# Four score tiles of head 1 brought forward ahead of head 0's last tile, with bias buffers of their own, and 24 identity turns behind them

## The reference, cut to what matters

```python
scores = q @ k.T / sqrt(64)
psi_rel = log1p(abs(pos[:, None] - pos[None, :])); psi_i = log1p(max(pos[:, None], 1))
bias = relu((psi_rel / psi_i)[..., None] @ w1 + b1) @ w2       # 576 x 576 x 8 heads
attn = softmax(scores + bias)
x = (attn @ v) of all heads as 2304 x 512
x = (s * relu(x @ w_in) ** 2 + b) @ w_out
out = (h - tanh(h)) @ w2_out, with h = x @ w2_in
```

## Time and profile before

| | |
|---|---|
| median of 3 runs | 1090.35 us (1090.28 to 1091.12) |
| the profiled execution, its own time | 1089.92 us |
| its span, first to last instruction | 1088.1 us |
| mean granted TensorE clock | 0.998 |
| busy: TensorE, VectorE, ScalarE, GpSimd | 97%, 57%, 67%, 63% |
| DMA, mean busy share by the queue of sync | 67.2% |

### The profile page before, as it was taken

One profiled execution on the slowest core, in us unless ns is written; L12 is line 12 of the kernel. 1 busy time (PEld: TensorE's weight loads), 2 busy tenths in 40 slices (PEclk: granted clock), 3 DMA queues, 4 the chain that ended last, 5 costly groups with the idle time before them and its releaser, 6 DMA issues.

```text
span 1088.1 us, 16872 instructions
## 1 busy us (share of the span) xinstructions
PE 1050.2 (97%) x5685; PEld 912.5 (84%) x5685; DVE 625.1 (57%) x1128; ACT 728.4 (67%) x1469; POOL 690.6 (63%) x656
## 2 busy tenths in 40 slices
PE   6679999999999999999999999999999999999998
PEld 2168889888888888888888888888888888999998
DVE  7968877655775475567747755761450451440640
ACT  8978888767878587777758766873562553552652
POOL 1056666687778778868876887766454455455553
PEclk9999999999999999999999999999999999999999
DMA  5788867799889788998996799764333333333331
GB/s 191 252 251 261 269 196 175 198 253 230 211 214 259 205 210 237 238 212 196 255 268 164 184 274 245 186 145 134 106 116 98 99 115 125 119 121 101 96 122 64
DMA packets 185338, 201.19 MB, mean 185 GB/s; under 512 B 125811, under 2 KB 129829, under 8 KB 185253
## 3 DMA queue, kind: packets, MB, share of 16 engines
q1 hardware_dynamic: 185108, 200.04, 67.2%
q10 hardware_dynamic: 144, 0.07, 0.1%
HBM read 155.23 MB, written 15.64 MB: 157 GB/s over the span
## 4 chain that ended last, share of the span: by engine, by line
PE 70%; ACT 14%; issue 7%; DVE 6%; DMA 2%; POOL 1%; SPq 0%; DVEq 0%; ACTq 0%; POOLq 0%
PE ps_f L919 19%; PE ps_f L921 19%; PE ps_f L920 19%; ACT x_raw L345 2%; PE ps_o L555 2%; DVE g_buf L979 2%; PE ps_s L594 2%; ACT planes L642 2%; ACT gh L932 2%; DVE g_buf L982 2%; PE ps_s L595 1%; PE ps_o L558 1%; PE ps_o L570 1%; ACT ps_t L654 1%; ACT gh L936 1%
## 5 line engine op out<-in xcount | busy, mean ns | idle before, releaser
L876 POOL TENSOR_TENSOR wl<-w_raw,wh 128x512 fp32r<-128x512 f32 x318 | 418.3, 1320 | 255.9 <-ACT wh L869 254.8
L919 PE MATMUL ps_f<-gh,wh 128*128 128x464 f32 (+1 forms) x640 | 242.7, 379 | 2.3 <-DVE g_buf L979 1.7
L919 PE MATMUL ps_f<-xh,wh 128*128 128x464 f32 (+1 forms) x640 | 240.5, 376 | 0.6 <-DVE ptl L748 0.6
L921 PE MATMUL ps_f<-xh,wl 128*128 128x464 f32 (+1 forms) x640 | 237.4, 371 | 0.0
L920 PE MATMUL ps_f<-gl,wh 128*128 128x464 f32 (+1 forms) x640 | 237.4, 371 | 0.0
L921 PE MATMUL ps_f<-gh,wl 128*128 128x464 f32 (+1 forms) x640 | 237.2, 371 | 0.0
L920 PE MATMUL ps_f<-xl,wh 128*128 128x464 f32 (+1 forms) x640 | 237.1, 370 | 0.0
L869 ACT ACTIVATE wh<-w_raw 128x512 fp32r<-128x512 f32 x318 | 196.6, 623 | 48.4 <-PE ps_f L921 48.2
L919 PEld LDWEIGHTS ps_f<-gh,wh 128*128 128x128 f32 x640 | 120.8, 189 | 16.0 <-DVE g_buf L979 2.8
L919 PEld LDWEIGHTS ps_f<-xh,wh 128*128 128x128 f32 x640 | 120.5, 188 | 13.4 <-DVE ptl L748 0.8
L921 PEld LDWEIGHTS ps_f<-xh,wl 128*128 128x128 f32 x640 | 120.1, 188 | 13.4
(11 more groups left out here) (126 smaller groups left out, 1694.8 us busy)
## 6 DMA issues: line engine op xcount, KB each, us to landing
w_raw<-in_w_out SPq DMA_DIRECT2D x80, 512.0 KB, 3.6
w_raw<-in_w_in SPq DMA_DIRECT2D x79, 512.0 KB, 3.5
bias_t<-bias_flat SPq DMA_DIRECT2D x128, 288.0 KB, 4.0
bias_flat<-stage SPq DMA_DIRECT2D x36, 295.5 KB, 2.2
k_raw<-in_kt SPq DMA_DIRECT2D x32, 288.0 KB, 4.1
q_raw<-in_qt SPq DMA_DIRECT2D x32, 288.0 KB, 3.6
v_raw<-in_vt SPq DMA_DIRECT2D x22, 288.0 KB, 3.2
bias_t<-bias_flat SPq DMA_DIRECT2D x32, 144.0 KB, 4.3
```

Of the source, the lines that this page charges most:

```text
L876: pool.tensor_tensor(wl[:, b % RING, :, :], raw_block(b), wh[:, b % RING, :, :].bitcast(F32), ALU.subtract).then_inc(w_lo_done, 1)
L919: pe.matmul(acc, hi, rhs_h[:, k0 + kk, 0:T], start=(first and kk == 0), stop=False)
L921: mm = pe.matmul(acc, lo, rhs_h[:, k0 + kk, 0:T], start=False, stop=(last and kk == 3))
```

## The change

Head 1's tiles 0 to 3 are scored, added and exponentiated in step 4, ahead of head 0's tile 4, and no longer in steps 5 to 8. Their bias goes to `early_bias`, four buffers which share their memory with `gl` (of the third stage), and is loaded right behind head 0's tile of the same t. The two banks go on alternating for these nine tiles. Sync then loads head 2's tiles 0 to 3 in steps 0 to 3 and nothing of the bias in steps 5 to 8. `neg_max` gets two halves by head. Head 1's q is rounded before step 0 and its low part taken at t = 0. The two weight blocks are rounded by ScalarE at g = 4 instead of 3, where GpSimd's low parts stay at g = 3. Behind step 4 TensorE does 24 turns of the identity into `ps_f`.

```diff
+PRE = 4
         def load_bias(sp, t):
...
             sp_bias(sp, 0, t)
+            if t < PRE:
+                sp_bias(sp, 1, t)
...
+        def scored_ahead(g):
+            if NT <= g < NT + PRE:
+                return g - 1
+            return NT + PRE - 1 if g == NT - 1 else g
+        def all_scored(n):
+            return NT + PRE if n == 0 else (n + 1) * NT
+        def scoring_at(g):
+            return g < TILES and not NT <= g < NT + PRE
         def score_bank(n, t):
-            if n == 0 and t % 2:
-                return ps_o
+            if n * NT + t < NT + PRE:
+                return ps_o if scored_ahead(n * NT + t) % 2 else ps_s
...
-            if n == 0:
-                need(pe, min_done, t - 1)
-                pe.wait_ge(back_done, PACKS - 2 if t == 0 else PACKS)
+            if n * NT + t < NT + PRE:
+                need(pe, min_done, scored_ahead(n * NT + t) - 1)
+                pe.wait_ge(back_done, PACKS - 2 if n + t == 0 else PACKS)
...
         def pe_turn(pe, i, alone):
             if t == 0:
-                pe.wait_ge(exp_done, (v + 1) * NT)
+                pe.wait_ge(exp_done, all_scored(v))
...
-            if t == 1 and n + 1 < BH:
+            if t == 1 and 0 < n < BH - 1:
                 act_round_q(act, n + 1)
...
-            if t == 1 and n + 1 < BH:
+            if t == (1 if n else 0) and n + 1 < BH:
                 pool_low_q(pool, n + 1)
...
         def sp_step(sp, g):
-            if n + 1 < BH:
-                sp.wait_ge(min_done, n * NT + t + 1)
-                sp_bias(sp, n + 1, t)
+            to = n + 1 if t >= PRE or n > 1 else 2 if n == 0 else BH
+            if to < BH:
+                sp.wait_ge(min_done, scored_ahead(g) + 1)
+                sp_bias(sp, to, t)
...
         @block.scalar
+            act_round_q(act, 1)
             for g in STEPS_AT[:FIRST]:
+                if g == NT - 1:
+                    for pre in range(NT, NT + PRE):
+                        act_exp(act, pre)
                 act_step(act, g, True)
-                if g == 3:
+                if g == NT - 1:
                     act_weights(act, 0)
                     act_weights(act, 1)
...
         @block.vector
+                if g == NT - 1:
+                    for pre in range(NT, NT + PRE):
+                        dve_add(dve, pre)
...
         @block.tensor
             for g in STEPS_AT[:FIRST]:
+                if g == NT - 1:
+                    for pre in range(NT, NT + PRE):
+                        pe_score(pe, *divmod(pre, NT))
+                if g == NT + PRE:
+                    pe.wait_ge(inv_row_done, 1)
                 pe_step(pe, g, True)
+                if g == NT - 1:
+                    pe_idle_turns(pe, ps_f, 24)
```

More of the change, by code:

```diff
@@ L123, in build @@
         v_loaded = sem("v_loaded")
+        early_loaded = [sem(f"early_loaded{i}") for i in range(PRE)]
         bias_loaded = [sem(f"bias_loaded{t}") for t in range(NT)]
@@ L200, in act_round_q @@
             act.wait_ge(q_loaded, (n + 1) * DMA)
-            need(act, s_done, (n - 1) * NT)
+            need(act, s_done, all_scored(n - 2) if n > 1 else 0)
             act.activation(q2[:, n % 2, 0:S], q_raw[:], ACT.Copy, scale=lower[:, 0:1]).then_inc(q_hi_done, 1)
@@ L205, in pool_round_k @@
             pool.wait_ge(k_loaded, (n + 1) * DMA)
-            need(pool, s_done, (n - 1) * NT)
+            need(pool, s_done, all_scored(n - 2) if n > 1 else 0)
             pool.tensor_copy(k2h[:, n % 2, :], k_raw[:]).then_inc(k_hi_done, 1)
@@ L217, in pool_low_k, with bias_home, bias_in @@
                 .then_inc(k_lo_done, 1)
+        def bias_home(n, t):
+            return early_bias[:, t, :] if n == 1 and t < PRE else bias_t[:, t, :]
+        def bias_in(eng, n, t):
+            if t >= PRE:
+                eng.wait_ge(bias_loaded[t], (n + 1) * DMA)
+            elif n == 1:
+                eng.wait_ge(early_loaded[t], DMA)
+            else:
+                eng.wait_ge(bias_loaded[t], max(n, 1) * DMA)
         def sp_bias(sp, n, t):
@@ L221, in sp_bias @@
             rows = bias_skew[P * t:P * t + R, bass.ds(n % H * PITCH + (S - 1), S)]
-            sp.dma_start(bias_t[0:R, t, :], rows).then_inc(bias_loaded[t], DMA)
+            loaded = early_loaded[t] if n == 1 and t < PRE else bias_loaded[t]
+            sp.dma_start(bias_home(n, t)[0:R, :], rows).then_inc(loaded, DMA)
         vhl = tile("vhl", [P, 2, NT, 2 * D], F32R)
@@ L230, in build @@
         o_tmp = tile("o_tmp", [D, 2, HALF])
-        neg_max = tile("neg_max", [P, NT])
+        neg_max = tile("neg_max", [P, 2, NT])
         den = tile("den", [P, 2, NT])
@@ L248, in build @@
         gh = tile("gh", [P, KF, TMAX], F32R)
+        with nc.sbuf_tensor("early_bias", [P, PRE, S], F32) as early_bias:
+            pass
         with nc.sbuf_tensor("gl_head", [P, KF - 2, TMAX], F32), nc.sbuf_tensor("p_odd", [P, S], F32) as p_odd:
@@ L620, in pe_step @@
                 pe_turn_inv(pe, n - 1)
-            if scoring(n):
+            if scoring_at(g):
                 pe_score(pe, n, t)
@@ L643, in act_plane, with act_exp @@
                 .then_inc(p_hi_done, 1)
+        def act_exp(act, g):
+            n, t = divmod(g, NT)
+            if t == 0:
+                need(act, den_done, min(n - 1, TURNED))
+            act.wait_ge(min_done, scored_ahead(g) + 1)
+            p = score_home(n, t)
+            act.activation(p, p, ACT.Exp, scale=-1.0, bias=neg_max[:, n % 2, t:t + 1],
+                           accum_out=den[:, n % 2, t:t + 1]).then_inc(exp_done, 1)
         def act_step(act, g, alone, between=None):
@@ L647, in act_step @@
             i, j = turned(g), valued(g)
[L649 to L655, removed]
             if j is not None and j % NT == NT - 1:
@@ L663, in act_step @@
                 act_plane(act, f)
-            if scoring(n) and alone and t == NT - 1:
-                exponential()
+            if scoring_at(g) and alone and t == NT - 1:
+                act_exp(act, g)
             if i is not None:
@@ L673, in act_step @@
                 between()
-            if scoring(n) and not (alone and t == NT - 1):
-                exponential()
+            if scoring_at(g) and not (alone and t == NT - 1):
+                act_exp(act, g)
             if n >= TURNED and between:
@@ L684, in act_step @@
                 need(act, inv_done, v)
-                act.wait_ge(exp_done, (v + 1) * NT)
+                act.wait_ge(exp_done, all_scored(v))
                 act.activation(den_e[:], den[:, v % 2, :], ACT.Copy, bias=1e-9).then_inc(den_done, 1)
-            if t == 1 and n + 1 < BH:
+            if t == 1 and 0 < n < BH - 1:
                 act_round_q(act, n + 1)
@@ L761, in dve_plane, with dve_add @@
                 .then_inc(p_lo_done, 1)
+        def dve_add(dve, g):
+            n, t = divmod(g, NT)
+            dve.wait_ge(s_done, scored_ahead(g) + 1)
+            bias_in(dve, n, t)
+            if t == 0 and n < TURNED:
+                need(dve, pt_done, (n - 1) * NT)
+            dve.tensor_tensor_reduce(out=score_home(n, t), in0=score_bank(n, t)[:, :, 0:HALF],
+                                     in1=halves(bias_home(n, t)), scale=-SCALE, scalar=3.0e38,
+                                     op0=ALU.add, op1=ALU.min, accum_out=neg_max[:, n % 2, t:t + 1])\
+                .then_inc(min_done, 1)
         def dve_step(dve, g, alone, between=None):
@@ L768, in dve_step @@
                 dve_scale(dve, f)
-            if scoring(n):
-                dve.wait_ge(s_done, g + 1)
+            if scoring_at(g):
+                dve.wait_ge(s_done, scored_ahead(g) + 1)
             if t == 3 and turning(n):
@@ L775, in dve_step @@
                 dve.tensor_copy(inv_row[:], ps_s[0:NT, 0, HALF:HALF + P]).then_inc(inv_row_done, 1)
[L776 to L783, removed]
+            if scoring_at(g):
+                dve_add(dve, g)
             if f is not None:
```

## The result

The changed kernel takes 1093.05 us (median of 22 runs, 1089.94 to 1096.59) against 1090.53 (22 runs of the kernel before, 1088.78 to 1092.49). The ratio is 1.0023, 95% interval 1.0018 to 1.0029. That is 2.5 us, just past the 0.2% that I had called distinguishable, and outside the range that I gave. The profiled execution took 1092.78 us with a span of 1091.0.

The account below looks back on a forecast made before the run. TensorE was taken to bound the steady stretch, DMA waits the passage. The q wait takes the offered 3.6 us, so (2,0) starts at 77.0 against 76.64: +0.4 on 1090.35, rounded to 1090.8 us; range 1088.7 to 1092.1.

Parts of the forecast that it names:

- The early loads in the tables: Table stage: three early bias loads between stores hidden to within 0.1 us, at most 1 us lost; put at 0.
- The load in front of the last stores: End of the tables: tile (1,3)'s load delays the last store and (0,4)'s bias by 0.8 us, bounds 0 to 1.0.
- Scores and additions in the gap: Passage to attention: four head 1 tiles fit into the bias wait, hiding 3.3 us, clock staying at 2.4 GHz.
- The 24 turns at 0.11 each, hidden: Behind step 4: turns take 2.6 us, ending at 68.7 before the first real turn at 68.75, costing nothing.
- ScalarE's wait for head 2's q: Step 6: q lands at 73.6, ScalarE waits 2.4 us, and the offered 3.6 us are gone.
- The shift stays: From head 2's first score on, the TensorE-bound loop carries the passage's +0.4 us to the end.
- Rival (c): Table stage: stalled stores hold ScalarE up some 0.6 us at each of three places, +1.8 us, 1092.6; 5%.
- (a): Passage: head 2's q comes soon enough, four shorter steps pay, (2,0) starts at 74 to 74.5, 1088.0 us; 12%.
- (b): Behind step 4: turns at 0.21 us each end at 71.1 and the slow clock holds on, +2.5, 1092.9 us; 5%.
- (d): Passage: the gap is merely filled, everything after stands as before, 1090.4 us; counted inside the forecast's 78%.

Follow-up runs that it names:

- Run 1: The kernel before plus only the change's bias buffers and early loads of head 1's tiles 0 to 3, no reordered scoring or turns: 1093.48 us, ratio 1.0026.
- run 3: The changed kernel without the 24 turns: 1093.07 us, ratio 1.0025.
- run 4: The changed kernel with head 2's k and q issued right behind bias (0,4), ahead of head 2's bias tiles: 1090.98 us, ratio 1.0003.
- Run 6: The changed kernel with only three tiles of head 1 loaded and scored ahead, so no load in front of the last two stores: 1092.25 us, ratio 1.0018.
- run 2: The changed kernel without its four early loads; head 1's first four tiles take head 0's bias: 1090.72 us, ratio 1.0005.
- run 10: The kernel of run 2 with head 2's k and q also issued right behind bias (0,4): 1089.71 us, ratio 0.9992.
- run 12: The kernel of run 9 without the 24 turns: 1092.66 us, ratio 1.0016.
- run 5: The changed kernel with head 1's bias tiles 0 to 2 loaded four packs behind head 0's and tile 3 behind bias (0,4): 1093.33 us, ratio 1.0030.
- run 8: The kernel of run 5 with head 2's k and q also issued early, after tile 3: 1093.26 us, ratio 1.0025.
- run 7: The kernel before with only head 2's k and q issued right behind bias (0,4), ahead of head 1's bias tiles: 1092.48 us, ratio 1.0019.
- run 9: The changed kernel with three early loads, four packs later, head 1's k and q at packs 11 and 15, head 2's behind bias (0,4): 1090.45 us, ratio 0.9997.

## Why the prediction was wrong

I forecast +0.4 us and 1090.8; it is +2.5 and 1093.05. By the steps of the prediction:

- **The early loads in the tables, "I put 0": this step failed.** I had written that the first place is hidden to within 0.1 us and priced the excess as a rival at 5%. The profile shows 0.6 us lost at pack 14, 0.3 at pack 22 and 0.2 at pack 30, 1.0 in all (tables 51.74 against 50.74), and 1.6 to 2.4 us in the profiles of runs 1, 3, 4 and 6, which have the same three loads. The four profiles with the old loads in the tables spread over 0.5 us, so the 1.0 of this one is rough, but the waits for the stage buffer name the place. The arithmetic missed two things, both seen at the first place: the store behind two loads lands after 4.4 us and not 3.2 + 0.9 = 4.1, and sync issues it 0.25 us later (25.36, less the 0.13 by which this execution ran late anyway, against 24.98), because issuing the extra load takes 0.47 us. Together 1.2 + 0.25 = 1.45 us against the slack of 0.9 (29.10 less 24.98 + 3.2): 0.55 us, as measured. With a slack that near zero, 0 was the lower bound and not the likeliest value; I should have carried some tenths at each of the three places. Run 1 shows the loads responsible; run 2 shows that the rest of the change costs nothing that the medians can tell.
- **The load in front of the last stores, 0.8 us: right mechanism, sized too low.** It measured 1.2 us (6.0 less 4.8 us from the last copy to the issue behind the last store), above my upper bound of 1.0. Run 6, with this load gone, has 5.1. As run 10 lost as much there without such a load, the size rests on single profiles; leaving run 10 out, they put it between 0.3 and 1.8 us.
- **Scores and additions in the gap: right.** (0,4)'s matmuls end at 67.46, 8.0 us after the last copy (7.7 worked out), and the clock is 1.00 where it was 0.50.
- **The 24 turns at 0.11 each, hidden: right.** They take 2.78 us from 67.30 to 70.08, just before the first real turn at 70.37. Run 3 shows no difference between the medians.
- **ScalarE's wait for head 2's q: right.** 2.83 us against the 2.4 foretold: counted from the last copy, q landed 0.6 us later than in the sum (0.4 of it from the last store), and ScalarE came free 0.2 later. (2,0) starts 0.84 us later from the last copy, where the sum had 0.4; mostly the same 0.4. Run 4 shows that this wait was the bound: it gives 2.1 us back. In run 2 the passage is as long as before, so the wait swallowed the whole gain.
- **"The shift stays": nearly.** (2,0) is 2.0 us late and the first feed-forward matmul 2.4 (154.27 against 151.88). That further 0.4 is a term that the sum put at nothing; all ten kernels that score ahead take longer there than the four that don't. Its cause stays open. The remaining 0.5 us of the profile's 2.9 lies in the third stage, inside the spread between executions.

Rival (c) was the right one in kind. It was not given its due because I asked it for the whole distance, +1.8 from the tables, while 1.0 from the tables and 0.8 from the passage do the same together. The other three cases fell: (a) since q took 5.4 us from its issue, as before, and came sooner only when run 4 moved its place in the list, (b) since the turns took 2.78 us with the granted clock at 1.00, (d) by the time itself.

How the three losses in the tables split between sync's later issue and the longer landing was worked out only at the first place; why the same loads cost 1.0 us in one profile and 2.4 in another is not settled.

## What to carry to other kernels

A transfer that is moved "into idle DMA time" has to be set against the slack of every buffer that is drained by the same queue: look up how long the nearest drain takes beside one load, and when its buffer is next written, and treat a slack near zero as a cost. Before filling a gap, look for the next wait behind it: here work was put into the first DMA wait while the second, for the next head's q, landed 6.7 us further on (72.8 against 66.1 in the kernel before), and moving two issues in sync's list gave back 2.1 of the 2.5 us that the change had lost. Even so, with every repair the kernel was no faster than before by more than its interval. Cover work, such as the turns, is worth little while a longer wait stands behind it. And a repair is judged by the medians: stretches of single profiles differed by 0.5 us and more between kernels that were alike there.

## What the runs showed of the hardware

- Stores of 295.5 KB landed after 3.2, 3.0 and 2.8 us behind one load of 288 KB at the three places of the kernel before, and after 4.4, 4.4 and 4.6 us behind two: 1.2 to 1.8 us for the second load, more than the 0.9 of the first at the first place. In the profiles of runs 2 and 10, with one load, they took 2.7 to 3.8 us, and in those of runs 1 and 4, with two, 4.0 to 4.7.
- TensorE's granted clock fell to 0.50 after 2.28 us of idle time in run 12 and 2.86 us in run 3, where the kernel before had been idle for 4.3 us; in runs 5 and 8 it was down to 0.50 after waits of only 1.81 and 1.99 us. With 24 turns in the same place and nothing else on TensorE it stayed at 1.00, so turns held the clock up here. The Trainium skill, page "TensorE: Matmul & The Clock Gate", section "Part 4: PE-mode transpose", says that transposes don't count as a busy TensorE in the same way; these runs go against it.
- The changed kernel's runs spread more widely, 1089.9 to 1096.6 us over 22 runs, against 1088.8 to 1092.5 before. That it is the early loads isn't shown: run 7, without them, spread from 1090.2 to 1095.8 us, and run 9, with three of them, from 1088.8 to 1091.5.
